# Three weight products of a MoE by Strassen's algorithm, in a kernel of attention and two MoEs

## The chip, the cores and the metric

One core of a Trainium2 chip. The metric is the device time of one execution in microseconds, as the median of several.

## The reference

```python
# attention: q, k, v of (4, 8, 576, 64); a banded and a downsampled softmax attention, summed
x = attn_out.transpose(0, 2, 1, 3).reshape(2304, 512)
h = x @ w_in                                   # first MoE, d_ff 2048
x = (h * np.clip(h + 3.0, 0.0, 6.0) / 6.0) @ w_out
h = np.maximum(np.maximum(x @ w1, x @ w2), x @ w3)   # second MoE, d_ff 768
return h @ w_out2                              # (2304, 512), float32
```

## The kernel before

The attention works on 16 pairs of heads (4 batches times 4 pairs). Pairs 4 to 15 are spread over the steps of the first MoE: `FIRST` (L145) gives the half-step at which each begins, and the last one ends at half-step 92, which is step 46.

Every product of the MoEs is made of three matmuls (`three`, L686): an operand is split into a high part (rounded to the matmul's format by a ScalarE copy) and a low part (operand minus high, by VectorE or GpSimd), and high x high, high x low and low x high are added in PSUM.

The first MoE takes the 2304 tokens in chunks of 512, 512, 512, 512 and 256 (`E1`, L126) and d_ff in 16 blocks of 128, which makes 80 steps; step s is chunk s // 16, block s % 16. In step s TensorE runs `hidden(s + 1)` (12 matmuls into bank 3) and then `add_out(s)` (12 matmuls into four banks). ScalarE and VectorE take each hidden block through `gate_relu`, `gate`, `gate_high` and `gate_low` (L1093, L1380, L1102, L1387). All engines run one program written out in order: what stands behind a waiting instruction on its engine waits with it. `hidden(s)` waits for `gate(s - 1)`, since there is one bank; `add_out(s)` waits for `gate_low(s)`. At a chunk's end `copy_y` (L1108 ScalarE, L1394 VectorE) takes the four result banks to y, and `store_y` (L482) sends y to a scratch tensor in HBM; the next chunk's first `add_out` waits for `copy_y`, bank by bank.

The second MoE has the same chunks (`E2`, L133). `load_xr` (L488) fetches a chunk of x, and `split_x2` (L1114, L1400) splits it, for chunk 0 in steps 56 to 59. A step `hidden2(e, f)` (L871) makes the three products of one block of 128 of the d_ff, 36 matmuls into three banks; there are two sets of three banks. `act_step2` (L1209) and `dve_step2` (L1469) take the maximum of the three and split it into hs. After a chunk's six steps `out2` (L966) multiplies hs with the last weight, 18 matmuls of 512 columns for each tile of 128 tokens, and `copy_out` (L1225) and a store take the result away. The four weights are loaded by `load_w2` (L498) into the places of the first MoE's weights, one after the other as its last chunk (steps 64 to 79) frees them, and split there by `high_w2` (L1125, ScalarE) and by GpSimd's subtraction (L678). Two thirds of `hidden2(0, 0)` stand ahead of `add_out(79)`, and the last third behind it.

DMAs are issued on SyncE's queue, in the order written, each behind its own waits.

## Time and profile before

| | |
|---|---|
| median of 3 runs | 809.03 us (808.30 to 810.23) |
| the profiled execution | 810.8 us, span 809.0 us |
| TensorE busy | 793.4 us, 98% of the span |
| VectorE, ScalarE, GpSimd busy | 314.1, 277.3, 164.1 us |
| HBM traffic | 38.79 MB read, 9.44 MB written |

The span runs from the first to the last instruction. A busy TensorE means that matmuls are in flight; they are pipelined, so one of 0.39 us may start 0.23 us after the one before it. The distance between two starts (the pitch) is therefore what a matmul costs in a stream. A view of groups says how long an instruction takes; the timeline says when it starts and, in brackets, for how long its engine was idle and what ended that.

### The profile page before, as it was taken

The page shows a single profiled execution, that of the slowest core. Times are in us where ns is not written, and L with a number is a line of the kernel's source. Part 1 is how long each engine was busy: PE and PEld are TensorE (multiplying, and loading weights), DVE is VectorE, ACT ScalarE, POOL GpSimd, SP SyncE. Part 2 cuts the span into 40 slices and gives each one's busy share as a digit, 9 for nine tenths or more (in the row PEclk, how much of TensorE's full clock was granted, in tenths as well). Part 3 has the DMA queues.
Part 4 walks back from the last instruction along what each step waited for, and adds up shares of the span by engine and source line. Part 5 has one row for each costly group of instructions (what it writes and reads, how often), then busy time and mean ns, then how long its engine had stood idle before and what let it go on. Part 6 is the DMA issues. An engine that isn't in the chain of part 4 may idle for free.

```text
span 809.0 us, 12700 instructions
## 1 busy us (share of the span) xinstructions
PE 793.4 (98%) x5344; PEld 659.0 (81%) x5344; DVE 314.1 (39%) x602; ACT 277.3 (34%) x619; POOL 164.1 (20%) x196
## 2 busy tenths in 40 slices
PE   7889999999999999999999999999999999999998
PEld 5667877888787878788888899888888888888897
DVE  5864556355444554553323334232123123112211
ACT  4745555343343434433223256221112112111111
POOL 7855756221022102210000048100000000000000
PEclk9999999999999999999999999999999999999999
DMA  8982412221211321110200066100110020010010
GB/s 176 207 260 69 113 48 61 57 79 39 62 39 32 103 62 32 30 32 30 76 1 0 1 196 188 61 0 1 53 52 1 36 70 0 14 66 0 14 40 27
DMA packets 93477, 49.06 MB, mean 61 GB/s; under 512 B 61164, under 2 KB 84204, under 8 KB 93420
## 3 DMA queue, kind: packets, MB, share of 16 engines
q1 hardware_dynamic: 90740, 47.36, 21.3%
q10 hardware_dynamic: 2680, 0.89, 0.6%
q8 instruction: 42, 0.69, 0.4%
q14 instruction: 15, 0.12, 0.1%
HBM read 38.79 MB, written 9.44 MB: 60 GB/s over the span
## 4 chain that ended last, share of the span: by engine, by line
PE 93%; POOL 2%; DVE 2%; ACT 1%; DMA 1%; SPq 1%; issue 1%; DVEq 0%; POOLq 0%
PE bank L688 29%; PE bank L690 28%; PE bank L689 28%; PE bank L823 1%; PE bank L800 1%; PE bank L745 1%; PE bank L789 1%; PE bank L762 1%; DMA k_nat_c<-in_k_dram 1%; PE bank L775 1%; POOL w L641 1%; PE bank L707 1%; POOL dp_a L633 1%; PE bank L717 1%; SPq L415 0%
## 5 line engine op out<-in xcount | busy, mean ns | idle before, releaser
L688 PE MATMUL bank<-xs,w 128*128 128x512 f32 (+1 forms) x680 | 253.5, 373 | 1.1 <-DVE xs L1356 1.0
L689 PE MATMUL bank<-xs,w 128*128 128x512 f32 (+1 forms) x680 | 250.5, 368 | 0.0
L690 PE MATMUL bank<-xs,w 128*128 128x512 f32 (+1 forms) x680 | 250.4, 368 | 0.0
L688 PEld LDWEIGHTS bank<-xs,w 128*128 128x128 f32 x680 | 128.4, 189 | 23.4 <-POOL w L641 1.4
L690 PEld LDWEIGHTS bank<-xs,w 128*128 128x128 f32 x680 | 128.3, 189 | 21.7
L689 PEld LDWEIGHTS bank<-xs,w 128*128 128x128 f32 x680 | 128.4, 189 | 20.4
L688 PE MATMUL bank<-gs,w 128*128 128x512 f32 (+1 forms) x320 | 121.6, 380 | 0.0
L1384 DVE SCALAR_TENSOR_TENSOR rg<-rg,bank 128x512 f32<-128x512 f32 (+1 forms) x80 | 50.7, 634 | 177.3 <-ACT rg L1100 177.3
L689 PE MATMUL bank<-gs,w 128*128 128x512 f32 (+1 forms) x320 | 118.1, 369 | 0.0
L690 PE MATMUL bank<-gs,w 128*128 128x512 f32 (+1 forms) x320 | 118.0, 369 | 0.0
L1100 ACT ACTIVATE rg<-bank,half 128x512 f32<-128x512 f32 (+1 forms) x80 | 51.6, 646 | 177.8 <-PE bank L690 177.8
L1391 DVE TENSOR_TENSOR gs<-rg,gs 128x512 fp32r<-128x512 f32 (+1 forms) x80 | 61.6, 770 | 39.2 <-ACT gs L1106 39.1
L1474 DVE TENSOR_TENSOR hm<-hm,bank 128x512 f32<-128x512 f32 (+1 forms) x30 | 19.0, 635 | 136.9 <-ACT hm L1215 136.9
L688 PEld LDWEIGHTS bank<-gs,w 128*128 128x128 f32 x320 | 60.3, 188 | 12.0 <-issue 1.9
L690 PEld LDWEIGHTS bank<-gs,w 128*128 128x128 f32 x320 | 60.3, 189 | 10.5
L689 PEld LDWEIGHTS bank<-gs,w 128*128 128x128 f32 x320 | 60.4, 189 | 8.9
L1215 ACT ACTIVATE hm<-bank 128x512 f32<-128x512 f32 (+1 forms) x30 | 16.7, 555 | 140.1 <-PE bank L690 140.1
L1106 ACT ACTIVATE gs<-rg 128x512 fp32r<-128x512 f32 (+1 forms) x80 | 47.3, 591 | 31.3 <-DVE rg L1384 31.3
L641 POOL TENSOR_TENSOR w<-w_raw,w 128x256 fp32r<-128x256 f32 x64 | 47.2, 768 | 28.4 <-ACT w L1072 28.4
L678 POOL TENSOR_TENSOR w<-w_raw,w 128x1024 fp32r<-128x1024 f32 x12 | 28.9, 2411 | 116.3 <-ACT w L1128 116.3
L1479 DVE TENSOR_TENSOR hs<-hm,hs 128x512 fp32r<-128x512 f32 (+1 forms) x30 | 19.2, 639 | 79.4 <-ACT hs L1223 79.4
L623 POOL TENSOR_TENSOR lp_a<-lp_a,linv_a 128x320 f32<-128x320 f32 x28 | 20.2, 741 | 145.8 <-DVE linv_a L1323 145.8
(211 smaller groups left out, 822.5 us busy)
## 6 DMA issues: line engine op xcount, KB each, us to landing
w_raw<-in_moe_w_out_dram SPq DMA_DIRECT2D x22, 256.0 KB, 4.8
w_raw<-in_moe_w_dram SPq DMA_DIRECT2D x18, 256.0 KB, 3.2
out_dram<-o_sb SPq DMA_DIRECT2D x18, 256.0 KB, 2.0
w_raw<-in_moe_w_in_dram SPq DMA_DIRECT2D x16, 256.0 KB, 3.9
x_scratch<-y SPq DMA_DIRECT2D x4, 1024.0 KB, 4.8
xr<-x_scratch SPq DMA_DIRECT2D x4, 1024.0 KB, 6.4
q_nat_a<-in_q_dram SPq DMA_DIRECT2D x26, 144.0 KB, 2.8
v_a<-in_v_dram SPq DMA_DIRECT2D x24, 144.0 KB
```

The costliest lines, as they stand in the source:

```text
L623: mine = g.tensor_tensor(lp[:, a:b], lp[:, a:b], t.linv[:, a:b].unsqueeze(2).to_broadcast([P, b - a, KW]), ALU.mult)
L641: mine = g.tensor_tensor(w1[:, f, 1, 2 * i:2 * i + 2], w1_raw[f][:, 2 * i:2 * i + 2], w1[:, f, 0, 2 * i:2 * i + 2].bitcast(F32), ALU.subtract)
L678: g.tensor_tensor(w2[:, m, 1], w2_raw[m][:], w2[:, m, 0].bitcast(F32), ALU.subtract).then_inc(s_w2, 1)
L688: mm(dst, w[0], m[0], start=start, stop=False, skip_group_check=True)
L689: mm(dst, w[0], m[1], start=False, stop=False, skip_group_check=True)
L690: return mm(dst, w[1], m[0], start=False, stop=stop, skip_group_check=True)
L1100: fn(gated(s), hidden_bank(s)[:, 0:n], ACT.Relu, bias=half[:, 0:1], scale=1.0 / 6.0).then_inc(s_relu, 1)
L1106: fn(gs[:, s % 2, 0, 0:n], gated(s), ACT.Copy).then_inc(s_gh, 1)
L1384: vec.scalar_tensor_tensor(out=gated(s), in0=gated(s), scalar=1.0, in1=hidden_bank(s)[:, 0:n], op0=ALU.min, op1=ALU.mult).then_inc(s_g, 1)
L1391: vec.tensor_tensor(gs[:, s % 2, 1, 0:n], gated(s), gs[:, s % 2, 0, 0:n].bitcast(F32), ALU.subtract).then_inc(s_gl, 1)
L1474: vec.tensor_tensor(got, got, bank[HBANK[f % 2][1]][:, 0:n], ALU.max).then_inc(s_m1, 1)
L1479: vec.tensor_tensor(hs[:, f, 1, 0:n], got, hs[:, f, 0, 0:n].bitcast(F32), ALU.subtract).then_inc(s_hl, 1)
```

## The change

The tokens of the second MoE are taken in three chunks of 768, and each of its three weights in three pieces of 256 columns (a pair of d_ff blocks). A block is one piece of one weight: a product of (768 x 512) with (512 x 256). Cut in two along each dimension it has eight products of quarters; Strassen's algorithm in Winograd's form has seven, of 384 tokens by 256 by 128, with four sums on either side and seven afterwards. Four sums of the weights' quarters (`sum_block`, VectorE), their high and low parts (`high_block` on ScalarE, `low_block` on GpSimd) are made after steps 47, 52, 53, 55, 56, 58, 59, 61 and 62 of the first MoE (`READY`) and stored to a new HBM tensor t2, 1.8 MB for each of nine blocks. There is one landing place b_raw for the weights and two sets of ph and pl for their parts. SyncE loads block b + 1 when block b's copies of b_raw are made, then stores block b. In the second MoE the blocks come back through a ring of four places, four of them (the last of the chunk before, in reversed order) without a load in chunks 1 and 2. The sums of x are made by `sum_x2`, `high_x2` and `low_x2`: for chunk 0 in steps 71 to 75, for the others during `out2`. Of the seven products, some are added up in PSUM (two banks take products 0 and 3 or 1 and 4, the third 2 and 5; product 6 takes the first again); the rest is added by VectorE, and one sum by GpSimd. The last weight is loaded and split by itself (`load_wo`, `high_wo`, `low_wo`).

The diff, cut to its core:

```diff
-    E2 = [0, 512, 1024, 1536, 2048, 2304]
-    NC2 = len(E2) - 1
-    N2 = [b - a for a, b in zip(E2, E2[1:])]
-    CH2 = max(N2)
-    T2 = [n // P for n in N2]
...
+    NC2 = 3
+    E2 = TOK // NC2
+    N2 = E2 // 2
+    T2 = E2 // P
+    PAIRS2 = F2 // 2
...
+    ORDER = [list(range(BLOCKS))[::1 - 2 * (e % 2)] for e in range(NC2)]
...
+    PRODUCTS = [0, 4, 3, 1, 5, 2, 6]
+    NPR = len(PRODUCTS)
+    RING = 4
...
+    LOADS = [(e, j) for e in range(NC2) for j in range(0 if e == 0 else RING, BLOCKS)]
...
+        READY = {47: 0, 52: 1, 53: 2, 55: 3, 56: 4, 58: 5, 59: 6, 61: 7, 62: 8}
+        BANKS2 = [[5, 6, 7], [0, 1, 2]]
...
+            def load_block(b):
+                if b == 0:
                     sp.wait_ge(s_x, 2 * NP)
                 else:
-                    sp.wait_ge(s_x2l, KT * e)
-                done = next(c for c in range(NC1) if E1[c + 1] >= E2[e + 1]) + 1
-                sp.wait_ge(s_ys, 16 * done)
-                sp.dma_start(xr[:, :, 0:N2[e]], x1[:, :, E2[e]:E2[e + 1]]).then_inc(s_xr, 16)
-            def load_w2(m):
-                sp.wait_ge(s_o, F1 * (NC1 - 1) + m + 1)
+                    sp.wait_ge(s_t, 4 * b)
+                    sp.wait_ge(s_th, 3 * b)
+                    sp.wait_ge(s_tl2, NPR * (b - 1) + 3)
+                sp.dma_start(b_raw[:].rearrange("p i k f c -> p (i k) (f c)"),
+                             w2_v[b % 3][b // 3]).then_inc(s_braw, 16)
+            def store_block(b):
+                sp.wait_ge(s_tl2, NPR * (b + 1))
+                for j, part_of in enumerate((ph, pl)):
+                    sp.dma_start(t2[b, :, j, :], part_of[b % 2][:].rearrange("p o k c -> p (o k c)").bitcast(F32)).then_inc(s_ts[b % 2], 16)
+            def load_xr(e):
+                if e:
+                    sp.wait_ge(s_xol, NPR * e)
+                done = next(c for c in range(NC1) if E1[c + 1] >= E2 * (e + 1)) + 1
+                sp.wait_ge(s_ys, 16 * max(done, NC1 - 1))
+                sp.dma_start(xr[:], x1[:, :, E2 * e:E2 * (e + 1)]).then_inc(s_xr, 16)
...
+            def load_wo(f):
                 for i in range(2):
-                    sp.dma_start(w2_raw[m][:, i * KT:(i + 1) * KT, :],
-                                 w2_v[2 * (m % 2) + i][m // 2]).then_inc(s_w2raw[m], 16)
+                    sp.wait_ge(s_ts[i], 32 * ((BLOCKS + 1 - i) // 2))
+                sp.dma_start(wo_raw[f][:], wo_v[f]).then_inc(s_wo[f], 16)
+            def load_wt(e, j):
+                b = ORDER[e][j]
+                i = b % RING
+                if j < RING:
+                    sp.wait_ge(s_o, F1 * (NC1 - 1) + NPR + 2 * i + 2)
+                else:
+                    sp.wait_ge(s_pr, NPR * (block2(e, j)[0] - RING + 1))
+                sp.wait_ge(s_ts[b % 2], 32 * (b // 2 + 1))
+                sp.dma_start(wt[i][:, :, 0:NPR].rearrange("p j o k c -> p j (o k c)").bitcast(F32), t2[b]).then_inc(s_wt[i], 16)
...
+            load_block(0)
             store_y(2)
+            for b in range(BLOCKS):
+                if b + 1 < BLOCKS:
+                    load_block(b + 1)
+                store_block(b)
+            store_y(3)
             load_xr(0)
-            store_y(3)
-            for m in range(2 * F2):
-                load_w2(m)
+            for f in range(F2):
+                load_wo(f)
+            for j in range(RING):
+                load_wt(0, j)
             load_xr(1)
...
             store_y(4)
+            for j in range(RING, BLOCKS):
+                load_wt(0, j)
             for e in range(NC2):
-                if e >= 1 and e + 1 < NC2:
-                    load_xr(e + 1)
-                for m in range(T2[e]):
-                    sp.wait_ge(s_oc, tile0(e) + m + 1)
...
+            def low_block(b):
+                high, low = ph[b % 2], pl[b % 2]
+                if b >= 2:
+                    pool.wait_ge(s_ts[b % 2], 32 * (b // 2))
+                for o, raw in enumerate((b_raw[:, 0, :, 0], b_raw[:, 1, :, 0], b_raw[:, 1, :, 1])):
+                    pool.wait_ge(s_th, 3 * b + 1 + o // 2)
+                    g.tensor_tensor(low[:, o], raw, high[:, o].bitcast(F32), ALU.subtract).then_inc(s_tl2, 1)
+                pool.wait_ge(s_t, 4 * b + 4)
+                pool.wait_ge(s_th, 3 * b + 3)
+                for o in range(3, NPR):
+                    g.tensor_tensor(low[:, o], pl_sum[b % 2][:, o], high[:, o].bitcast(F32),
+                                    ALU.subtract).then_inc(s_tl2, 1)
+            for b in range(BLOCKS):
+                low_block(b)
...
+            def sum_c22(e, j):
+                t, i, w = block2(e, j)
+                pool.wait_ge(s_v, t + 1)
+                pool.wait_ge(s_p5, t + 1)
+                if j % 3 == 0:
+                    if t:
+                        pool.wait_ge(s_hl, 4 * (t // 3 - 1) + 2)
+                    g.tensor_tensor(hm[3], v_t[:], p5[:], ALU.add).then_inc(s_c22, 1)
+                else:
+                    g.tensor_tensor(p5[:], v_t[:], p5[:], ALU.add).then_inc(s_add, 1)
+            for e in range(NC2):
+                for j in range(BLOCKS):
+                    sum_c22(e, j)
+                    if e == 0 and 1 <= j < 1 + F2:
+                        low_wo(j - 1)
...
+            def product(e, j, i):
+                t, _, _ = block2(e, j)
+                b = ORDER[e][j]
+                if j == 0:
+                    pe.wait_ge(s_xol, NPR * e + i + 1)
+                if i == 0:
+                    pe.wait_ge(s_wt[b % RING], 16 * loads_of(e, j))
+                    if t >= 2:
+                        pe.wait_ge(s_c21, t - 1)
+                    if t == 1:
+                        pe.wait_ge(s_yv, 2 * NC1)
+                        pe.wait_ge(s_ya, 2 * NC1)
+                if i == 3:
+                    pe.wait_ge(s_p1, t + 1)
+                if i == 4:
+                    pe.wait_ge(s_u2, t + 1)
+                if i == 5:
+                    pe.wait_ge(s_p5, t + 1)
+                if i == 6:
+                    pe.wait_ge(s_c11, t + 1)
+                dst = bank[BANKS2[t % 2][i % 3]][:, 0:N2]
+                for kk in range(2):
+                    mine = three(dst, [wt[b % RING][:, h, PRODUCTS[i], kk, :] for h in range(2)],
+                                 [xo[i][:, h, kk, :] for h in range(2)],
+                                 kk == 0 and i in (0, 1, 2, 6), kk == 1)
+                mine.then_inc(s_pr, 1)
             def add_out(s):
...
                 add_out(s)
                 attend(2 * s + 1)
-            OBANK = [4, 7]
...
-                    if m == 0 or f0:
-                        pe.wait_ge(s_hl, F2 * e + f + 1)
-                    whi, wlo = (w2[:, 2 * f + 1, j, KT:2 * KT, :].rearrange("p a b -> p (a b)") for j in range(2))
-                    mine = three(bank[OBANK[i % 2]][:], [hs[:, f, j, m * P:(m + 1) * P] for j in range(2)],
-                                 [whi, wlo], f == 0, f == F2 - 1)
-                if f1 == F2:
+                for at in range(a, b):
+                    pe.wait_ge(s_hl, 4 * (PAIRS2 * e + at) + 3 + (at < PAIRS2 - 1 or m >= T2 // 2))
+                    if e == 0:
+                        pe.wait_ge(s_wol, F2)
+                    pair = ORDER[e][3 * at] // 3
+                    for x in range(2):
+                        mine = three(bank[OBANK[i % 2]][:], [hs[pair][:, x, h, m * P:(m + 1) * P] for h in range(2)],
+                                     [wo[:, 2 * pair + x, h] for h in range(2)], at == 0 and x == 0,
+                                     at == PAIRS2 - 1 and x == 1)
+                if b == PAIRS2:
                     mine.then_inc(s_o2, 1)
-            hidden2(0, 0, (0,))
-            pe.wait_ge(s_yv, 2 * NC1)
-            pe.wait_ge(s_ya, 2 * NC1)
+            for i in range(3, NPR):
+                product(0, 0, i)
             for e in range(NC2):
-                for f in range(1, F2):
-                    hidden2(e, f)
...
-                    for m in range(T2[e]):
-                        out2(e, m, 0, F2 - 1)
-                    for m in range(T2[e]):
-                        out2(e, m, F2 - 1, F2)
+                for j in range(0 if e else 1, BLOCKS):
+                    for i in range(NPR):
+                        product(e, j, i)
+                for m in range(2):
+                    out2(e, m, 0, PAIRS2 - 1)
+                for m in range(2):
+                    out2(e, m, PAIRS2 - 1, PAIRS2)
+                for m in range(2, T2):
+                    out2(e, m, 0, PAIRS2)
...
+            def high_block(b):
+                high, low = ph[b % 2], pl_sum[b % 2]
+                act.wait_ge(s_braw, 16 * (b + 1))
+                if b >= 2:
+                    act.wait_ge(s_ts[b % 2], 32 * (b // 2))
+                fn(high[:, 0:2], b_raw[:, :, :, 0], ACT.Copy).then_inc(s_th, 1)
+                fn(high[:, 2], b_raw[:, 1, :, 1], ACT.Copy).then_inc(s_th, 1)
+                act.wait_ge(s_t, 4 * b + 4)
+                fn(high[:, 3:NPR], low[:, 3:NPR], ACT.Copy).then_inc(s_th, 1)
+            def high_x2(e, i):
+                if i == 0:
                     act.wait_ge(s_xr, 16 * (e + 1))
-                if e == 1:
-                    act.wait_ge(s_ys, 16 * (NC1 - 1))
-                if e >= 2:
-                    act.wait_ge(s_h2, F2 * (e - 1))
-                fn(xs2[e % 2][:, 0, kk, 0:N2[e]], xr[:, kk, 0:N2[e]], ACT.Copy).then_inc(s_x2h, 1)
...
-                act.wait_ge(s_w2raw[m], 32)
-                fn(w2[:, m, 0], w2_raw[m][:], ACT.Copy).then_inc(s_w2h, 1)
+                if e:
+                    act.wait_ge(s_pr, NPR * BLOCKS * e)
+                else:
+                    act.wait_ge(s_o, F1 * (NC1 - 1) + i + 1)
+                if i in (1, 2, 4, 5):
+                    act.wait_ge(s_s, 4 * e + {2: 1, 1: 2, 4: 3, 5: 4}[i])
+                    src = xo_sum[i][:]
+                else:
+                    src = {0: xr[:, 0:2, 0:N2], 3: xr[:, 2:4, 0:N2], 6: xr[:, 2:4, N2:E2]}[i]
...
-                if c == NC1 - 2 and 8 <= f < 12:
-                    split_x2(0, f - 8)
-                if c == NC1 - 1 and 2 <= f < 2 + 2 * F2:
-                    high_w2(f - 2)
+                if s in READY:
+                    high_block(READY[s])
+                if c == NC1 - 1 and 7 <= f < 11:
+                    for i in range(NPR)[2 * (f - 7):2 * (f - 6)]:
+                        high_x2(0, i)
                 if f == F1 - 1:
...
-                for f in range(F2):
-                    act_step2(e, f)
-                    if 1 <= f < 5 and e + 1 < NC2:
-                        split_x2(e + 1, f - 1)
-            copy_out(NC2 - 1)
+                for j in range(BLOCKS):
+                    copy_p1(e, j)
+                    if j and j % 3 == 0:
+                        high_h(e, j - 1, 3)
+                        high_h(e, j - 1, 1)
+                    copy_p5(e, j)
+                    if j and j % 3 == 0:
+                        high_h(e, j - 1, 2)
+                    if j % 3 == 2:
+                        high_h(e, j, 0)
+                    if e == 0 and j < F2:
+                        high_wo(j)
+                for which in (3, 1, 2):
+                    high_h(e, BLOCKS - 1, which)
...
+            def sum_block(b):
+                low = pl_sum[b % 2]
+                dve.wait_ge(s_braw, 16 * (b + 1))
+                if b >= 2:
+                    dve.wait_ge(s_ts[b % 2], 32 * (b // 2))
+                t1, t2, t3, t4 = (low[:, 3 + i] for i in range(4))
+                b11, b12, b21, b22 = (b_raw[:, i, :, j] for i in range(2) for j in range(2))
+                vec.tensor_tensor(t1, b12, b11, ALU.subtract).then_inc(s_t, 1)
+                vec.tensor_tensor(t3, b22, b12, ALU.subtract).then_inc(s_t, 1)
+                dve.wait_ge(s_t, 4 * b + 1)
+                vec.tensor_tensor(t2, b22, t1, ALU.subtract).then_inc(s_t, 1)
+                dve.wait_ge(s_t, 4 * b + 3)
+                vec.tensor_tensor(t4, b21, t2, ALU.subtract).then_inc(s_t, 1)
...
+            def sum_x2(e):
+                dve.wait_ge(s_xr, 16 * (e + 1))
...
+                    dve.wait_ge(s_pr, NPR * BLOCKS * e)
+                else:
+                    dve.wait_ge(s_o, F1 * (NC1 - 1) + NPR)
+                s2, s1, s3, s4 = (xo_sum[i][:] for i in (1, 2, 4, 5))
+                a11, a12, a21, a22 = (xr[:, j:j + 2, i * N2:(i + 1) * N2] for i in range(2) for j in (0, 2))
+                vec.tensor_tensor(s1, a21, a22, ALU.add).then_inc(s_s, 1)
+                dve.wait_ge(s_s, 4 * e + 1)
+                vec.tensor_tensor(s2, s1, a11, ALU.subtract).then_inc(s_s, 1)
+                vec.tensor_tensor(s3, a11, a21, ALU.subtract).then_inc(s_s, 1)
+                dve.wait_ge(s_s, 4 * e + 2)
+                vec.tensor_tensor(s4, a12, s2, ALU.subtract).then_inc(s_s, 1)
...
+            def low_x2(e, i):
+                dve.wait_ge(s_xoh, NPR * e + i + 1)
+                if i in (1, 2):
+                    dve.wait_ge(s_s, 4 * e + 4)
+                src = {0: xr[:, 0:2, 0:N2], 3: xr[:, 2:4, 0:N2], 6: xr[:, 2:4, N2:E2]}.get(i)
+                src = xo_sum[i][:] if src is None else src
+                vec.tensor_tensor(xo[i][:, 1], src, xo[i][:, 0].bitcast(F32), ALU.subtract).then_inc(s_xol, 1)
...
+                if s in READY:
+                    sum_block(READY[s])
+                if c == NC1 - 1 and f == 7:
+                    sum_x2(0)
+                if c == NC1 - 1 and 8 <= f < 12:
+                    for i in range(NPR)[2 * (f - 8):2 * (f - 7)]:
+                        low_x2(0, i)
                 if f == F1 - 1:
...
-                for f in range(F2):
-                    dve_step2(e, f)
-                    if 1 <= f < 5 and e + 1 < NC2:
-                        split_x2(e + 1, f - 1)
+                for j in range(BLOCKS):
+                    take_u2(e, j)
...
+                        low_h(e, j - 1, 3)
+                    take_c11(e, j)
+                    if j and j % 3 == 0:
+                        low_h(e, j - 1, 1)
+                        low_h(e, j - 1, 2)
+                    take_v(e, j)
+                    take_c12(e, j)
+                    if j % 3:
+                        max_c12(e, j)
+                        max_c22(e, j)
+                    take_c21(e, j)
+                    if j % 3:
+                        max_c21(e, j)
+                for which in (0, 3, 1, 2):
+                    low_h(e, BLOCKS - 1, which)
+                if e + 1 < NC2:
+                    sum_x2(e + 1)
+                    for i in range(NPR):
+                        low_x2(e + 1, i)
```

## Rows read from the trace of the kernel before

**Rows 1.** The page: the span, section 1 of TensorE, the granted clock of section 2.
```profile
span 809.0 us, 12700 instructions
...
PE 793.4 (98%) x5344; PEld 659.0 (81%) x5344; DVE 314.1 (39%) x602; ACT 277.3 (34%) x619; POOL 164.1 (20%) x196
...
PEclk9999999999999999999999999999999999999999
```
**Rows 2.** Busy time by stretch: us, PE, PEld, DVE, ACT, POOL (x), PEclk, DMA share, GB/s.
```profile
700.00:740.00 40.00, 40.00 (x178) 33.14 (x177) 6.10 (x11) 6.58 (x12) 0.00 (x0) 1.00 0.12 40
```
**Rows 3.** Timeline of ScalarE, chunk 0 of the second MoE; start us, us, instruction.
```profile
526.97 0.60 ACT L1215 ACTIVATE hm<-bank 128x512 f32<-128x512 f32 x1 [5.45 <-PE bank L690]
...
535.13 0.60 ACT L1215 ACTIVATE hm<-bank 128x512 f32<-128x512 f32 x1 [4.93 <-PE bank L690]
```
**Rows 4.** Timeline of ScalarE, last chunk of the first MoE.
```profile
504.84 0.47 ACT L1100 ACTIVATE rg<-bank,half 128x256 f32<-128x256 f32 x1 [0.55 <-PE bank L690]
...
507.72 0.47 ACT L1100 ACTIVATE rg<-bank,half 128x256 f32<-128x256 f32 x1 [0.55 <-PE bank L690]
```
**Rows 5.** Timeline of TensorE: `hidden(79)`'s last matmul, the second MoE's first and last.
```profile
507.40 0.28 PE L690 MATMUL bank<-xs,w 128*128 128x256 f32 x1
...
508.96 0.40 PE L688 MATMUL bank<-xs,w 128*128 128x512 f32 x1
...
805.46 0.39 PE L690 MATMUL bank<-w,hs 128*128 128x512 f32 x1
```
**Rows 6.** Groups by line and shape (busy us, mean ns, idle before), one timeline row.
```profile
L1479 DVE TENSOR_TENSOR hs<-hm,hs 128x512 fp32r<-128x512 f32 x24 | 16.6, 693 | 61.0 <-ACT hs L1223 61.0
...
L1479 DVE TENSOR_TENSOR hs<-hm,hs 128x256 fp32r<-128x256 f32 x6 | 2.6, 426 | 18.4 <-ACT hs L1223 18.4
...
L1128 ACT ACTIVATE w<-w_raw 128x1024 fp32r<-128x1024 f32 x12 | 12.5, 1044 | 0.1
...
L1223 ACT ACTIVATE hs<-hm 128x512 fp32r<-128x512 f32 x24 | 15.2, 632 | 31.0 <-DVE hm L1476 31.0
...
L1223 ACT ACTIVATE hs<-hm 128x256 fp32r<-128x256 f32 x6 | 2.5, 416 | 4.7 <-DVE hm L1476 4.7
...
L1015 ACT ACTIVATE kT_a<-bank 128x384 f32<-128x384 f32 x14 | 7.0, 501 | 0.0
...
516.06 0.66 ACT L1112 ACTIVATE y<-bank 128x256 f32<-128x256 f32 x2 [6.96 <-PE bank L690]
```
**Rows 7.** Timeline of ScalarE and VectorE, last step of 512 columns.
```profile
459.07 0.69 ACT L1100 ACTIVATE rg<-bank,half 128x512 f32<-128x512 f32 x1 [3.36 <-PE bank L690]
460.51 0.63 ACT L1106 ACTIVATE gs<-rg 128x512 fp32r<-128x512 f32 x1 [0.76 <-DVE rg L1384]
...
459.79 0.69 DVE L1384 SCALAR_TENSOR_TENSOR rg<-rg,bank 128x512 f32<-128x512 f32 x1 [3.36 <-ACT rg L1100]
461.18 0.69 DVE L1391 TENSOR_TENSOR gs<-rg,gs 128x512 fp32r<-128x512 f32 x1 [0.70 <-ACT gs L1106]
```
**Rows 8.** Timeline of GpSimd and VectorE where both work, in the first MoE.
```profile
127.62 2.82 POOL L641 TENSOR_TENSOR w<-w_raw,w 128x256 fp32r<-128x256 f32 x4 [5.74 <-ACT w L1072]
...
134.02 3.95 POOL L641 TENSOR_TENSOR w<-w_raw,w 128x256 fp32r<-128x256 f32 x4 [1.53 <-ACT w L1072]
...
134.76 1.22 DVE L1391 TENSOR_TENSOR gs<-rg,gs 128x512 fp32r<-128x512 f32 x1
...
480.34 1.03 DVE L1391 TENSOR_TENSOR gs<-rg,gs 128x256 fp32r<-128x256 f32 x1 [0.48 <-ACT gs L1106]
...
478.67 2.40 POOL L678 TENSOR_TENSOR w<-w_raw,w 128x1024 fp32r<-128x1024 f32 x1 [0.69 <-ACT w L1128]
```
**Rows 9.** DMA issues (KB each, median us from issue to landing); one stretch of an xr load.
```profile
xr<-x_scratch SPq DMA_DIRECT2D x4, 1024.0 KB, 6.4
...
xr<-x_scratch SPq DMA_DIRECT2D x1, 512.0 KB, 3.9
...
588.00:589.00 1.00, 1.00 (x6) 0.84 (x5) 0.00 (x0) 0.00 (x0) 0.00 (x0) 1.00 1.02 395
```

More of the change, by code:

```diff
@@ L311, in attention_moe_kernel @@
+        hm = [hm_a[:, 0], hm_a[:, 1], hm_b[:, 0], hm_b[:, 1]]
+        hs_at = [xs_at[0], xs_at[0] + 2 * 2 * E2 * 4, M_AT - W_FSZ]
+        hs = [place(hs_at[i], f"hs{i}", [P, 2, 2, E2], F32R) for i in range(PAIRS2)]
+        assert hs_at[1] + 2 * 2 * E2 * 4 <= gs_end and xs_at[1] + 4 * (KT * E2 + 2 * N2) <= xs_at[0]
+        assert hs_at[2] + 2 * 2 * E2 * 4 <= xs_at[1]
         q_v = q.rearrange("b h (j r) d -> b h r j d", j=J)
```

299 lines of the change are left out of this document (193 added, 106 removed).

## The prediction

> **What bounds the kernel now.** I read four views in this order. First the page: TensorE is busy for 98% of the span and its granted clock stands at the full level, 2.4 GHz, in every slice [rows 1]. So the question is what the matmuls cost and whether anything makes them wait. Second, the busy time by stretch: inside the second MoE TensorE is busy 40.00 of 40.00 us while VectorE and ScalarE are busy for about 6 us each [rows 2]. Third, the timeline, for the pitch of one matmul. Two ScalarE evictions of successive steps of the second MoE start 8.16 us apart [rows 3]; a step is 36 matmuls of 512 columns, so one takes 0.2267 us. Two steps of the first MoE's last chunk are 2.88 us apart for 24 matmuls of 256 columns [rows 4], 0.1200 us each. Both lie on one line: 0.0133 us and 0.4167 ns per column (2.4 GHz). For 384 columns, which no row has, the line gives 0.1733 us. Its bounds are 0.170 (proportional to 512) and 0.2267 (no cheaper than 512); I take the line, since two widths lie on it. Fourth, the ends: the second MoE's first matmul starts at 508.96, its last at 805.46 [rows 5]. Counting 1188 matmuls of 512, 216 of 256 and the 12 of the last `add_out` gives 269.3 + 25.9 + 1.4 = 296.6 us; the rows leave 296.5 + 0.2. There is no stall in the second MoE, so each matmul removed is time won and each new wait is time lost.
>
> **What is removed.** The products with three weights are 864 matmuls of 512 and 216 of 256: 195.8 + 25.9 = 221.8 us. After: 3 chunks x 9 blocks x 7 products x 2 x 3 = 1134 of 384 columns, 196.6 us. `out2` stays at 324 of 512. **Gain 25.2 us.**
>
> At this place the Trainium skill, "TensorE: Matmul & The Clock Gate", section "Back-to-back issue gap", speaks against the change: it gives about 131 ns per matmul sustained at 512 columns and 81 ns at 128, so that narrow matmuls cost nearly what wide ones do. Interpolated, an estimate, the gain would be 5 us. The pitches of [rows 3, 4] contradict it.
>
> **Inside the new second MoE.** A product is six matmuls, 1.04 us; a block is 7.28 us. VectorE does up to 8 operations per block and 4 more per pair, 0.56 us each (between 0.426 at 256 and 0.693 at 512 columns, [rows 6]): 4.5 us of 7.28. ScalarE adds two evictions of 0.50 us and GpSimd one sum of about 1.05 us (0.70 per 256 columns, [rows 8]). A result is taken up 0.20 us after its last matmul gives way to the next (507.40 + 0.12, eviction at 507.72; [rows 4, 5]). So p1 is there at 1.8 us and wanted at 3.1; u2 at 2.9, wanted at 4.2; p5 at 3.9, wanted at 5.2; c11 at 5.0, wanted at 6.2. VectorE's last maximum ends near 9.4 and the next block's u2 can start at 9.6. Every margin is over 1 us, so I cost these waits at nothing; if VectorE fell behind by 1.3 us per block it would be the bound. A block's weights are 1.8 MB; at the 395 GB/s of a full stretch [rows 9] that is 4.7 us plus a start of about 1.4, and only five loads per chunk fall into 58 us. Nothing.
>
> Four places are not covered:
> - Start: ScalarE must copy y(4) (0.66 us for two, [rows 6]) after the last `add_out`, then p1, before product 3: 0.2 + 0.66 + 0.5 = **1.4 us**. Before, `hidden2` covered this.
> - Ends of chunks 0 and 1: `copy_out(e,0)` stands behind `high_x2` 1 and 2, which wait for VectorE's sums, which stand behind four `low_h`. I get the copy at 15.9 us after the last product, against TensorE's 15.4: 0.5 us, twice, **1.0 us**.
> - The first chunk's operands, made in steps of 2.88 us. At f = 7 VectorE runs four sums of 768 columns (0.96 each by the line through [rows 6]) after `gate_low`, ending at 5.5 us, so the gate ends at 5.9 where `hidden` wants it at 4.1: 1.9. Then three steps with two `low_x2` take VectorE 3.2 us of 2.88: 0.9. **2.8 us.** GpSimd is idle then.
> - The weights' sums, made at the listed steps of the first MoE, 5.44 us each.
>
> **The weights' sums** are the large term. A step's chain begins with `gate_relu`; from it to the end of `gate_high` are 2.07 us and to the end of `gate_low` 2.80 (459.07, 460.51, 459.79, 461.18 and their lengths, [rows 7]). `high_block` and `sum_block` stand behind these, and the next `gate_relu` stands behind `high_block` on ScalarE. `hidden(s+2)` can begin 2.72 us after `hidden(s+1)` ends and wants the gate; with 0.69 + 0.03 + 0.69 + 0.05 us for relu and gate, `gate_relu` may be 1.06 us late at no cost. The last action of `high_block` (1024 columns, 1.05 us, [rows 6]) waits for VectorE's four dependent sums.
>
> Those compete with GpSimd's lows. The trace: four GpSimd subtractions take 2.82 us alone, but 3.95 when VectorE starts operations with two SBUF inputs beside them, one of which takes 1.22 us instead of 0.69; and a VectorE subtraction of 256 columns takes 1.03 instead of 0.43 when a GpSimd one of 2.40 is under way, ending with it [rows 8]. So they take turns. This is the rule of the Trainium skill, "SBUF — State Buffer", section "Who interferes with whom": a shared port, held for a whole instruction, and the loser blocks. By that rule the sum is the one below; without it, it is the first rival.
>
> First block of a pair (steps 52, 55, 58, 61), from relu = 0: GpSimd and VectorE alternate from 2.8 (0.67 and 0.30), the sums end at 6.2, `high_block` at 7.3; relu and gate end at 8.7 against 7.96: **0.8 us**. Only then is b_raw free. Its next load of 512 KB in 1 KB pieces takes 3.9 us like the xr load of that size [rows 9]: landed at 11.3. The second block (steps 53, 56, 59, 62) follows one step behind, so ScalarE sits in `high_block` with `gate_relu` behind it: two copies (0.63 + 0.4, [rows 6]), the sums and the last copy end 3.3 to 3.9 after landing, at 14.9; the gate at 16.35 against 14.2: **2.15 us**. Three pairs: **8.9**. The fourth runs into the 256-column chunk: 0.8 + 2.9, and 0.5 more because `copy_y(3)` is late: **4.2**. Block 0 at step 47 delays `copy_y(2)`: sums end at 6.2, the first copy at 6.9, `add_out(48)` wants it at 5.24, and ScalarE's copy adds 0.3: **1.9**. Bounds of this group (15.0): 8 (no turns, sums end early) and 25 (the load takes 6.4 us like the 1 MB one, four times 2.5 more).
>
> Each of some 17 stalls also shows a weight load that was hidden; loads are busy 659.0 us in 5344 [rows 1], 0.12 each: **2.0 us**. Removed work (`high_w2`, GpSimd's part of it, `split_x2`) lay beside TensorE and gives nothing.
>
> Sum: -25.2 + 1.4 + 1.0 + 2.8 + 15.0 + 2.0 = -3.0 us. The profiled execution took 810.8 (span 809.0), 1.8 above the median of 809.03; so 807.8 in a like execution, **806.0 us** as a median. A difference under 0.2% (1.6 us) can't be told from none.
>
> **Rivals.**
> 1. The cover holds better: VectorE's sums are not held up by GpSimd. Then first blocks cost nothing, second ones 1.4, the group 8: 799. For: the order of turns is only seen in few rows, and the first two sums may precede GpSimd's. Against: [rows 8]. Chance 0.25. That nearly no stall appears (786) has 0.05: it needs b_raw to land 3 us sooner than any such load here.
> 2. Slower: the reload of b_raw. It is issued alone and its landing decides four times. At 4.65 us instead of 3.9 the gain is gone; at 6.4, the 1 MB row, it is 10 us worse: 816. Against: stores of the block before are done by then by my count. Chance 0.15.
> 3. The new phase is bound by the blocks' weights: by the slope between the xr loads of 512 KB and 1 MB (3.9 and 6.4 us, [rows 9]) a block takes 10.1 us, more than its 7.28, and chunk 0, where nine must come, would lose about 5 us: 811. Against: the stretch with 395 GB/s. Chance 0.07.
> 4. It does not cut TensorE's time as counted: a 384-column matmul costs 0.20 us, halfway to the upper bound. Then 1134 x 0.027 = 30 us go, and 836 results. Against: the line through two widths. Chance 0.03. The interpolated rule of the Trainium skill's page on TensorE, above, is of this kind and would give about 826.
> The forecast keeps 0.45, its own range 802 to 810.
>
> **The numbers.** Range 795 to 814: it takes in the forecast, rival 1, rival 3 and half of rival 2. Faster: 0.27 of the forecast's 0.45, and 0.30, makes 0.57. Same: 0.13 and 0.05, 0.18. Slower: 0.25.
>
> **What would show it.** Evictions of the second MoE 7.28 us apart per block and matmuls of 384 columns 0.173 apart; in the list of waits TensorE waiting in the first MoE for the gate (VectorE), about 2 us at a time, with ScalarE's `high_block` waiting for the b_raw load just before; VectorE's sums of 256 columns lasting 0.7 to 0.8 us. If `gate_relu` of steps 55, 58 and 61 starts on time, the large term is wrong. If TensorE waits inside blocks for u2 or c11, or for weights by DMA, my margins are wrong.

## The result, and the profile after

The changed kernel takes **798.51 us** (median of four runs, 797.5 to 799.76), the kernel before 809.63 beside it (808.3 to 812.01): ratio 0.9867, 95% interval 0.9851 to 0.9883. The profiled execution took 799.48 us. It is faster, as forecast, and clear of the spread, but by 11 us and not by 3. The time lies inside the stated range of 795 to 814, close to rival 1's 799 and not to the forecast's 806.

The page of the kernel after, cut:

```profile
span 797.7 us, 13594 instructions
...
PE 773.2 (97%) x5398; PEld 668.3 (84%) x5398; DVE 414.9 (52%) x786; ACT 299.5 (38%) x671; POOL 221.7 (28%) x280
...
wt<-t_scratch SPq DMA_DIRECT2D x19, 1792.0 KB, 7.6
...
b_raw<-in_moe_w_dram SPq DMA_DIRECT2D x9, 512.0 KB, 3.8
```

Against [rows 1] TensorE is busy 20.2 us less in 54 matmuls more, and VectorE 101 us more. TensorE is still the bound; the question is how long it waits. Its list of waits (what was waited for: us in total, times, longest):

```profile
PE bank L841 <- DVE rg L1587: 7.1, 7, 1.8
...
PE bank L841 <- DVE y L1601: 1.3, 1, 1.3
PE bank L841 <- ACT p L1392: 1.2, 1, 1.2
```

The first is the gate of the first MoE, late seven times; the second is `copy_y(2)` at step 48; the third is the first product's copy when the second MoE starts. Nothing in the second MoE waits for a DMA or for VectorE. The timeline of TensorE shows its matmuls' pitch and two of the stalls:

```profile
420.64 0.50 PE L841 MATMUL bank<-xs,w 128*128 128x512 f32 x1 [1.16 <-DVE rg L1587]
...
474.43 0.39 PE L841 MATMUL bank<-xs,w 128*128 128x256 f32 x1 [1.83 <-DVE rg L1587]
...
521.31 0.34 PE L841 MATMUL bank<-xo,wt 128*128 128x384 f32 x1
521.48 0.34 PE L842 MATMUL bank<-xo,wt 128*128 128x384 f32 x1
...
794.15 0.39 PE L843 MATMUL bank<-wo,hs 128*128 128x512 f32 x1
```

A matmul of 384 columns starts 0.17 us after the one before. From 521.31 to 794.15 + 0.23 are 273.1 us, where the kernel before needed 296.7 [rows 5]: **23.6 us** won in the second MoE. By count it is 1134 x 0.1733 + 324 x 0.2267 + 1.4 (the last `add_out`) = 271.4; the wait at the start, another 1.4 us, and 0.3 of small gaps are the rest. In the timeline of ScalarE the blocks' first evictions stand 7.28 us apart, as counted:

```profile
532.72 0.49 ACT L1392 ACTIVATE p<-bank 128x384 f32<-128x384 f32 x1 [4.72 <-PE bank L843]
...
540.00 0.49 ACT L1392 ACTIVATE p<-bank 128x384 f32<-128x384 f32 x1 [4.19 <-PE bank L843]
```

**What the stalls cost.** For each stall I take the distance between two matmuls' starts less the pitch of their width, from TensorE's timeline. After 366 us, where the weights' sums begin, the kernel before loses 0.3 us so; the changed one:

| place | forecast | measured |
|---|---|---|
| block 0, step 48 | 1.9 | 1.5 |
| three first blocks of a pair | 2.4 | 0.9 |
| three second blocks | 6.45 | 3.7 |
| ahead of the 256-column chunk | 4.2 | 2.3 |
| chunk 0's operands | 2.8 | 2.1 |
| start of the second MoE | 1.4 | 1.4 |
| chunk ends | 1.0 | 0 |
| restarts, other small gaps | 2.0 | 1.3 |
| half clock behind one stall | 0 | 1.7 |
| sum | 22.2 | 14.9 |

A stall's restart is inside "measured" where it shows in the first gap; the second matmul comes another 0.1 us late, which the line on restarts holds. The gain of 25.2 less 14.9, with the 0.3 us of the kernel before, is 10.6. The profiled difference is 810.8 − 799.48 = 11.3, and 1.0 us of it is a first MoE that reached step 48 sooner, which differs between executions (375.2 to 377.8 us over ten profiles of these kernels). That leaves 10.3 for the change, so the table accounts for it within 0.3 us.

One pair of blocks, in the timeline of four engines, shows where the stall at 420.64 comes from:

```profile
405.40 0.69 ACT L1260 ACTIVATE rg<-bank,half 128x512 f32<-128x512 f32 x1 [3.06 <-PE bank L843]
...
411.33 1.06 ACT L1285 ACTIVATE ph<-pl_sum 128x1024 fp32r<-128x1024 f32 x1 [3.03 <-DVE pl_sum L1618]
412.30 0.67 ACT L1260 ACTIVATE rg<-bank,half 128x512 f32<-128x512 f32 x1
...
416.22 0.63 ACT L1281 ACTIVATE ph<-b_raw 128x512 fp32r<-128x512 f32 x1 [1.87 <-DMA b_raw<-in_moe_w_dram]
...
418.23 1.06 ACT L1285 ACTIVATE ph<-pl_sum 128x1024 fp32r<-128x1024 f32 x1 [1.07 <-DVE pl_sum L1618]
419.20 0.67 ACT L1260 ACTIVATE rg<-bank,half 128x512 f32<-128x512 f32 x1
...
408.12 0.97 DVE L1613 TENSOR_TENSOR pl_sum<-b_raw 128x256 f32<-128x256 f32 x1
409.01 0.95 DVE L1614 TENSOR_TENSOR pl_sum<-b_raw 128x256 f32<-128x256 f32 x1
409.89 0.95 DVE L1616 TENSOR_TENSOR pl_sum<-b_raw,pl_sum 128x256 f32<-128x256 f32 x1
410.88 0.42 DVE L1618 TENSOR_TENSOR pl_sum<-b_raw,pl_sum 128x256 f32<-128x256 f32 x1
...
416.22 0.43 DVE L1613 TENSOR_TENSOR pl_sum<-b_raw 128x256 f32<-128x256 f32 x1 [1.02 <-DMA b_raw<-in_moe_w_dram]
...
417.36 0.84 DVE L1618 TENSOR_TENSOR pl_sum<-b_raw,pl_sum 128x256 f32<-128x256 f32 x1
...
408.07 2.49 POOL L798 TENSOR_TENSOR pl<-b_raw,ph 128x256 fp32r<-128x256 f32 x3 [21.66 <-ACT ph L1281]
...
417.00 2.50 POOL L798 TENSOR_TENSOR pl<-b_raw,ph 128x256 fp32r<-128x256 f32 x3 [1.19 <-ACT ph L1281]
...
412.48 0.38 SPq L568 DMA_DIRECT2D b_raw<-in_moe_w_dram  x1
```

First block: `gate_relu` starts at 405.40. While GpSimd makes its three lows (408.07 to 410.56), VectorE's sums of 256 columns last 0.95 to 0.97 us; the fourth, with GpSimd done, 0.42. ScalarE waits 3.03 us in the middle of `high_block` for them, and the next `gate_relu` (412.30) is that late. Second block: the load goes out at 412.48, since it waits for all three copies of the first block, and lands at 416.22; ScalarE stands in `high_block` again, the next `gate_relu` can't start before 419.20, and TensorE stalls at 420.64. That is the forecast's chain. It is shorter than forecast because in the second block GpSimd begins 0.8 us after the landing and only the last sum is held up.

### The profile page after: what moved, and what is told of

Read it like the earlier page. It is cut to its first block, busy times and chain, and to the rows that moved or that the text cites. A ratio compares the mean times of both kernels' runs of the same rounds, so it can differ in the third digit from the quotient of the medians.

```text
span 797.7 us, 13594 instructions
## 1 busy us (share of the span) xinstructions
PE 773.2 (97%) x5398; PEld 668.3 (84%) x5398; DVE 414.9 (52%) x786; ACT 299.5 (38%) x671; POOL 221.7 (28%) x280
## 4 chain that ended last, share of the span: by engine, by line
PE 83%; DVE 5%; ACT 3%; POOL 3%; DMA 2%; SPq 2%; issue 2%; DVEq 0%; POOLq 0%
PE bank L841 26%; PE bank L843 25%; PE bank L842 25%; DMA b_raw<-in_moe_w_dram 2%; PE bank L976 1%; PE bank L953 1%; PE bank L898 1%; POOL w L755 1%; DVE rg L1587 1%; ACT rg L1260 1%; PE bank L942 1%; DVE pl_sum L1618 1%; PE bank L915 1%; PE bank L928 1%; DVE pl_sum L1616 1%
## 5 line engine op out<-in xcount | busy, mean ns | idle before, releaser
L841 PE MATMUL bank<-xs,w 128*128 128x512 f32 (+1 forms) x320 | 122.8, 384 | 8.2 <-DVE rg L1587 7.1
L841 PE MATMUL bank<-xo,wt 128*128 128x384 f32 x378 | 126.4, 334 | 1.2 <-ACT p L1392 1.2
L843 PE MATMUL bank<-xo,wt 128*128 128x384 f32 x378 | 126.3, 334 | 0.0
L842 PE MATMUL bank<-xo,wt 128*128 128x384 f32 x378 | 126.3, 334 | 0.0
L843 PE MATMUL bank<-xs,w 128*128 128x512 f32 (+1 forms) x320 | 118.6, 371 | 0.0
L842 PE MATMUL bank<-xs,w 128*128 128x512 f32 (+1 forms) x320 | 118.5, 370 | 0.0
L841 PEld LDWEIGHTS bank<-xs,w 128*128 128x128 f32 x320 | 60.7, 190 | 23.3 <-DVE rg L1587 10.2
L1594 DVE TENSOR_TENSOR gs<-rg,gs 128x512 fp32r<-128x512 f32 (+1 forms) x80 | 57.8, 723 | 39.2 <-ACT gs L1266 39.1
L841 PEld LDWEIGHTS bank<-xo,wt 128*128 128x128 f32 x378 | 70.9, 188 | 1.5 <-issue 1.4
L842 PEld LDWEIGHTS bank<-xo,wt 128*128 128x128 f32 x378 | 71.0, 188 | 0.1
L843 PEld LDWEIGHTS bank<-xo,wt 128*128 128x128 f32 x378 | 70.9, 188 | 0.0
L843 PEld LDWEIGHTS bank<-xs,w 128*128 128x128 f32 x320 | 60.7, 190 | 10.5
L842 PEld LDWEIGHTS bank<-xs,w 128*128 128x128 f32 x320 | 61.0, 190 | 9.0
```

What stands on the lines that cost most here:

```text
L841: mm(dst, w[0], m[0], start=start, stop=False, skip_group_check=True)
L842: mm(dst, w[0], m[1], start=False, stop=False, skip_group_check=True)
L843: return mm(dst, w[1], m[0], start=False, stop=stop, skip_group_check=True)
L1594: vec.tensor_tensor(gs[:, s % 2, 1, 0:n], gated(s), gs[:, s % 2, 0, 0:n].bitcast(F32), ALU.subtract).then_inc(s_gl, 1)
```

## The experiments

The question after the result is what the remaining 15 us hang on. **Theory A**: the reload of b_raw lands too late. **Theory B**: GpSimd and VectorE take turns, and ScalarE waits for the held-up sums. In the trace both stand in the same chain. The kernel before took 809.50 us beside the runs with the second b_raw, the load sooner, the wait on GpSimd and the one block, and 810.08 beside the others, so a difference of medians from the two groups is uncertain by some 0.6 us.

**A second b_raw**, loads two blocks ahead:

```diff
+        b_raws = [b_raw, work("b_raw1", [P, 2, 2, 2, P])]
...
-                else:
+                elif b >= 2:
-                    sp.wait_ge(s_t, 4 * b)
+                    sp.wait_ge(s_t, 4 * (b - 1))
...
-                if b + 1 < BLOCKS:
-                    load_block(b + 1)
+                if b + 2 < BLOCKS:
+                    load_block(b + 2)
```

> The landing place b_raw is doubled, so that a block's load is issued two blocks ahead. Theory A (the second block of a pair is late because ScalarE waits 1.8 us for b_raw's reload): the three stalls of 1.1 to 1.3 us and most of the one of 2.0 us before the 256-column chunk go; about 5 us less than the changed kernel, near 793.5. Theory B (VectorE and GpSimd take turns at a shared port): VectorE's sums can start 1 us sooner, but then each of the four meets GpSimd's subtractions of the block before and of its own and takes 0.95 us instead of 0.43, so they end no sooner; within 1 us of the changed kernel, near 798, with sums of 0.95 us in the trace.

Measured: 802.39 us, ratio to before 0.9903 [0.9886, 0.9921]: 4 us **slower** than the change as it was. Neither theory had that: A put it at 793.5, B at 798. Its list of waits has the gate late for longer:

```profile
PE bank L844 <- DVE rg L1591: 9.4, 7, 2.4
```

VectorE's timeline in the second block of the same pair:

```profile
416.23 0.96 DVE L1618 TENSOR_TENSOR pl_sum<-b_raw 128x256 f32<-128x256 f32 x1
...
418.98 0.84 DVE L1623 TENSOR_TENSOR pl_sum<-b_raw,pl_sum 128x256 f32<-128x256 f32 x1
```

The data is there; now the sums start while GpSimd is at its lows, and last 0.96, 0.96, 0.95 and 0.84 instead of 0.43, 0.42, 0.42 and 0.84. Counted from the `gate_relu` ahead of them (413.40 here, 412.30 in the change) the sums start 1.1 us sooner (at 2.83 and not 3.92) and end 0.5 us later (at 6.42 and not 5.90). The stall of a second block grows from 1.25 to 1.84 us. So B had the mechanism, and only its size too small.

**The same load, released one copy sooner** (ScalarE's last copy reads the sums, not b_raw):

```diff
-                    sp.wait_ge(s_th, 3 * b)
+                    sp.wait_ge(s_th, 3 * b - 1)
```

> The reload of b_raw waits for the two copies that read it and no longer for the third, which reads the sums: it is issued about 1.1 us sooner. If the second blocks' stalls are set by the landing (A), each of the three shrinks from about 1.25 to about 0.2 us and the last from 2.0 to 0.9: about 4.4 us less, near 794. If they are set by the turns of VectorE and GpSimd (B), the sums start sooner but meet GpSimd's last four subtractions of the block before (until 415.8 in the changed kernel's profile, the landing would be at 415.1): 1 to 2 us less, near 797.

Measured: 801.01 us, 0.9891 [0.9871, 0.9911], 2.5 us slower, where A had 794 and B 797. This interval overlaps the change's own (0.9851 to 0.9883); the profile says the same as the median, with 13.5 us of gaps against 11.6. The timelines of SyncE, VectorE and GpSimd:

```profile
410.08 0.38 SPq L568 DMA_DIRECT2D b_raw<-in_moe_w_dram  x1
...
413.88 0.96 DVE L1613 TENSOR_TENSOR pl_sum<-b_raw 128x256 f32<-128x256 f32 x1
...
416.63 0.84 DVE L1618 TENSOR_TENSOR pl_sum<-b_raw,pl_sum 128x256 f32<-128x256 f32 x1
...
411.29 3.27 POOL L804 TENSOR_TENSOR pl<-pl_sum,ph 128x256 fp32r<-128x256 f32 x4 [1.97 <-ACT ph L1285]
414.63 2.56 POOL L798 TENSOR_TENSOR pl<-b_raw,ph 128x256 fp32r<-128x256 f32 x3
```

Against ScalarE's last copy of the first block (410.09 here, 411.33 in the change) the load goes out 1.2 us sooner and the sums begin 1.1 us sooner (3.79 us behind it, not 4.89). They fall into the 3.27 us in which GpSimd still makes the block before, and then beside its three lows. The turns take back more than the landing gives: their four lengths are 3.7 us here and 2.1 in the change. Theory A alone is refuted twice: an earlier landing makes the stalls longer. Theory B's forecast of a small gain is missed too, since it counted the turns with the block before and not those with the block's own three lows.

**GpSimd's lows behind the sums**, one wait more on GpSimd:

```diff
+                pool.wait_ge(s_t, 4 * b + 4)
                 for o, raw in enumerate((b_raw[:, 0, :, 0], ...
```

> One wait more: GpSimd's first three subtractions of a block wait until VectorE's four sums of that block are made. Theory B (turns): all four sums take 0.43 us, they end 1.4 us sooner in first blocks and 0.4 in second ones; first-block stalls (0.24 to 0.39) go, the one at step 48 shrinks by 1.3, second ones by 0.8 each; about 5 us less, near 793.5. Theory A (only the reload counts): GpSimd's third subtraction, which frees b_raw, comes later or at the same time, so nothing is gained: 798 to 799.

Measured: 794.19 us, 0.9812 [0.9797, 0.9827], 4.3 us faster than the change. Its list of waits has the gate late five times, not seven:

```profile
PE bank L842 <- DVE rg L1588: 5.7, 5, 1.6
```

The timelines of VectorE (second block), GpSimd (first block) and SyncE:

```profile
414.11 0.43 DVE L1614 TENSOR_TENSOR pl_sum<-b_raw 128x256 f32<-128x256 f32 x1 [1.97 <-DMA b_raw<-in_moe_w_dram]
...
415.24 0.43 DVE L1619 TENSOR_TENSOR pl_sum<-b_raw,pl_sum 128x256 f32<-128x256 f32 x1
...
408.06 2.14 POOL L799 TENSOR_TENSOR pl<-b_raw,ph 128x256 fp32r<-128x256 f32 x3 [21.96 <-DVE pl_sum L1619]
...
410.30 0.38 SPq L568 DMA_DIRECT2D b_raw<-in_moe_w_dram  x1
```

No engine does less; it is the order. The four sums last 0.42 to 0.43 us each, GpSimd's three lows 2.14 instead of 2.49. The stall at step 48 and the three at first blocks are gone (2.4 us), the seconds fall from 1.25 to 1.0. What is left of them is the landing: the load goes out at 410.30, behind the lows that now come later, and lands at 414.11.

**Both**, the second b_raw and the wait:

> GpSimd's wait together with the doubled b_raw, which alone made it slower. Theory B (turns): now the second block's sums meet only GpSimd's last four subtractions of the block before, two sums take about 0.9 us and two 0.43, and they end 1 us sooner than with the wait alone; second-block stalls of 1.0 us go, the last one (1.75) shrinks to 0.7: about 790. Theory A (reload) by itself expects the same here, but did not expect the doubled b_raw alone to be slower. If the four late subtractions hold up all four sums, it is no faster than the wait alone: 794.

Measured: 790.23 us, 0.9757 [0.9741, 0.9773]. With the turns out of the way the second b_raw is worth 4.0 us, where it cost 3.9 without. Its list of waits shows the gate late twice, ahead of the 256-column chunk and at chunk 0's operands, and no more in any pair of the 512-column chunks:

```profile
PE bank L845 <- DVE rg L1592: 2.2, 2, 1.5
```

VectorE's first two sums of a second block still last 0.95 us there, beside GpSimd's four lows of the block before (409.67 to 413.13), but now they start early enough. So the two waits cover each other, and each theory is right about what is left once the other's wait is gone.

**One block instead of nine.** This kernel makes block 0's weights' sums only and reads them for all nine blocks, so eight of its nine blocks have the wrong weights:

```diff
-        READY = {47: 0, 52: 1, 53: 2, 55: 3, 56: 4, 58: 5, 59: 6, 61: 7, 62: 8}
+        READY = {47: 0}
...
-            for b in range(BLOCKS):
-                low_block(b)
+            low_block(0)
```

> Only block 0 of the weights' sums is made and stored, and the second MoE reads it for all nine: blocks 1 to 8 are left out. The stalls counted from the matmuls' starts say what they cost: 0.9 (first blocks) + 3.7 (second ones) + 2.3 (before the 256-column chunk) and up to 1.7 where the granted clock fell to half for 3.4 us: 7 to 9 us less, 790 to 791.5. If the eight blocks also cost something that those stalls do not show (traffic that slows the matmuls, a later start of the weights' loads), it is more than 9.

Measured: 790.63 us, 0.9762 [0.9747, 0.9777]. The eight blocks cost 7.9 us, all that they do to the second MoE's loads included; by the table they are 0.9 + 3.7 + 2.3 of stalls, restarts, and at times the clock. Step 48, the operands and the start stay (1.5, 1.7, 1.4). The kernel with both waits removed reaches 790.23 while it makes all nine.

**The three places outside the sums.** ScalarE's first product copy ahead of `copy_y(4)`; at step 47 `copy_y(2)` ahead of `high_block` and `sum_block`; VectorE's four sums of chunk 0 split over steps 71 and 72 and its `low_x2` over five steps, and ScalarE's `high_x2` over five steps and not four:

```diff
+                if s in READY and f == F1 - 1:
+                    copy_y(c)
                 if s in READY:
                     high_block(READY[s])
...
+                if s == STEPS - 1:
+                    copy_p1(0, 0)
...
-                if c == NC1 - 1 and f == 7:
-                    sum_x2(0)
+                if c == NC1 - 1 and f in (7, 8):
+                    sum_x2(0, f - 7)
```

> Three changes of place, nothing else: p1 of block 0 is copied ahead of y(4) on ScalarE; chunk 0's sums of x are made two per step (steps 71 and 72) and their low parts up to step 77, not four sums in one step; at step 47 both engines copy y(2) ahead of block 0 of the weights' sums. If the stalls of 1.38, 1.71 and 1.54 us stand for themselves, they go and the time falls by about 4.5 us, to 794. Rival: a stall taken away is given back by the next thing that is late (block 0's load or the low parts for product 6), and less than 2.5 us is gained.

Measured: 795.82 us, 0.9827 [0.9813, 0.9842], 2.7 us faster than the change, between the expected 4.5 and the rival's 2.5. The operands' stall is gone (1.7), the start falls from 1.38 to 0.52 and waits for VectorE's u2 now. At step 48 the copy is on time and the stall only moves: ScalarE's `high_block` now ends later, the gate of the next step with it (0.91 instead of 1.54).

**That order with the wait on GpSimd**, and **all three**:

> The three changes of place, and GpSimd's first three subtractions behind VectorE's sums. The waits lie at different places: 794.2 (GpSimd's wait alone) less 1.4 and 1.7, the one at step 48 being gone already: about 791. Rival: block 0 now ends later than before at step 48 and delays step 49: 793.

> Everything together: GpSimd's wait, doubled b_raw, three changes of place. No stall over 0.3 us is left but about 0.7 ahead of the 256-column chunk: 13.2 of the counted 15 us (and the fallen clock) are won back at the most; about 787, near the 786 that the count of matmuls alone gives. Rival: the doubled b_raw gives nothing beside GpSimd's wait: 791.

Measured: 791.93 us, 0.9778 [0.9763, 0.9792], and **787.80 us, 0.9729 [0.9715, 0.9744]** (787.35 to 789.12). The latter beats both kernels: 10.7 us below the change, 22.3 below the kernel before beside it. Its page:

```profile
span 786.1 us, 13596 instructions
...
PE 770.2 (98%) x5398; PEld 667.0 (85%) x5398; DVE 411.2 (52%) x786; ACT 300.0 (38%) x671; POOL 219.0 (28%) x280
```

From 366 us on its list of waits holds one late gate, the start and a wait for `copy_y(3)`:

```profile
PE bank L845 <- DVE rg L1597: 0.7, 1, 0.7
...
PE bank L845 <- DVE u L1738: 0.4, 1, 0.4
...
PE bank L845 <- DVE y L1611: 0.3, 1, 0.3
```

In gaps of over 0.12 us it loses 2.0 us there, of 25.2 that the removed matmuls give. The stalls and the medians, side by side:

| kernel | us | step 48 | first | second | 256 chunk | operands | start | gaps after 366 us |
|---|---|---|---|---|---|---|---|---|
| the change | 798.51 | 1.5 | 0.9 | 3.7 | 2.3 | 1.7 | 1.4 | 11.6 |
| second b_raw | 802.39 | 1.5 | 0.9 | 5.5 | 2.9 | 1.7 | 1.4 | 14.0 |
| load sooner | 801.01 | 1.5 | 0.9 | 5.6 | 2.4 | 1.7 | 1.4 | 13.5 |
| wait on GpSimd | 794.19 | 0 | 0 | 3.0 | 2.2 | 1.7 | 1.4 | 8.3 |
| order | 795.82 | 0.9 | 0.9 | 4.1 | 2.6 | 0 | 0.5 | 9.1 |
| wait, order | 791.93 | 0 | 0 | 2.7 | 2.2 | 0 | 0.5 | 5.4 |
| wait, second b_raw | 790.23 | 0 | 0 | 0 | 1.3 | 1.7 | 1.4 | 4.4 |
| all three | 787.80 | 0 | 0 | 0.1 | 1.3 | 0 | 0.5 | 2.0 |

The last column sums the gaps over 0.12 us, without the clock; chunk 0's operands are 1.7 here and 2.1 above, where the small gaps behind the long one count too. Medians and stalls agree step by step: the wait on GpSimd 3.3 us in gaps and 4.3 in the median (its profile has the full clock behind the stall ahead of the 256-column chunk, 1.00 from 470 to 476 us, where the change's fell), the second b_raw on top of it 3.9 and 4.0, the order on top of both 2.4 and 2.4.

## Why the prediction was right or wrong

The step that failed is the size of the weights' sums, the large term of the sum: 15.0 us forecast, 8.4 measured, 6.6 too many. Restarts (2.0 against 1.3), the chunk ends (1.0 against 0) and chunk 0's operands (2.8 against 2.1) were too large as well, 2.4 us together; a fall of the clock that the sum didn't have took 1.7 back. So the losses were 14.9 and not 22.2, against a gain that was right: 10.3 us are left where the forecast had 3, and the first MoE that came 1.0 us sooner makes it 11. The mechanism of the term holds, as the wait on GpSimd and the second b_raw show; what failed in it is how long the chain takes.

**The gain: right.** 25.2 us rested on the line through two widths; 384 columns have the pitch that it gives, 0.173 us, and blocks stand 7.28 apart. Rival 4 falls. The Trainium skill, "TensorE: Matmul & The Clock Gate", section "Back-to-back issue gap", gives about 0.131 us a matmul sustained at 512 columns, by which the estimated gain was 5 us. The traces contradict it, with 0.227 us at 512 columns and 0.173 at 384.

**Inside the second MoE: right.** No wait for u2, p5, c11 or a block's weights. The weights' loads take 7.6 us where the text had 4.7 plus 1.4, so that term was too small; against five loads in a chunk of 58 us it doesn't show: TensorE never waits for one. Rival 3, which had 10.1 us a load, falls with it.

**The start: right** (1.4 forecast, 1.38 measured), and the cure confirms what it waited for.

**The chunk ends: wrong, 1.0 us that isn't there.** The forecast had the copy at 15.9 against TensorE's 15.4. (It says "after the last product", but both figures count from the start of the last block, here 582.44.) ScalarE's row shows it from 14.4 to 15.0 us:

```profile
596.87 0.58 ACT L1424 ACTIVATE o_sb<-bank 128x512 f32<-128x512 f32 x1
```

The step that failed here is the price of the operations: I added whole lengths (0.56, 0.96). In a row of operations one starts before the last one's length is over: here the sums of 0.95 us stand 0.87 apart and operations on 384 columns, 0.55 long, 0.47; the sums at 409.01 and 409.89 above do the same. (A sum that needs the result of the one before comes later: 0.99 us here.) A length is what one operation takes, a pitch is what it costs in a row. I had used the pitch for the matmuls and the length for everything else.

**Chunk 0's operands: right place, 2.8 against 2.1.** The long stall is 1.7 where 1.9 stood; the three later steps cost some 0.1 us each and not 0.3, for the same reason.

**The weights' sums: right chain, size off by 6.6 us** (15.0 forecast, 8.4 measured, inside the bounds of 8 and 25). Block 0 is 0.4 of it, and three steps of the sum did the rest. (1) First blocks: relu and gate were put 0.8 us late; the sums ended at 5.9 us and `high_block` at 7.0, not 6.2 and 7.3, and 0.3 was left. (2) Second blocks: the load takes 3.7 us against 3.9, and with the sooner release it lands at 10.8 and not 11.3. But from the landing to the end of the last copy I had 3.3 to 3.9 and took the middle. Only the last of the four sums is held up, since GpSimd begins 0.8 us after the landing. It is 3.1 (416.22 to 419.29), `gate_relu` comes at 13.8 instead of 14.9, and the stall is 1.25 instead of 2.15. (3) Ahead of the 256-column chunk 2.3 instead of 4.2: each piece as in (1) and (2), and the 0.5 for `copy_y(3)` didn't appear. (With the wait on GpSimd it does: TensorE's first `add_out` of that chunk is 0.46 us late for VectorE's y.)

**Restarts: too large.** 0.12 us for each of 17 stalls stood there; some ten stalls came, each with 0.1 us at its second matmul.

**Rival 1**, "VectorE's sums are not held up", gave 799 and the time is 798.5. The time was met and the reason was not: in the changed kernel the sums of every first block are held up. The experiment with the wait on GpSimd is the case that rival 1 described, and it takes 794. What helped the number is that in second blocks three of the four sums come ahead of GpSimd's lows, as the rival said two might. Its group of 8 us has no stall in first blocks and 1.4 us in second ones, the measured 8.4 has 0.3 and 1.25. That the time then fell on 799 is luck: the terms outside the group were 2.4 us too large, and the clock, which no term had, took 1.7. A number that fits is no proof of its mechanism. The taking of turns is the rule that the prediction drew from the Trainium skill, "SBUF — State Buffer", section "Who interferes with whom"; the trace agrees with it: 0.95 us beside GpSimd, 0.43 without. The order that avoids most of it is worth 4.3 us of the kernel's time. One of its rows was read loosely: the subtraction that starts at 480.34 [rows 8] ends 0.3 us behind GpSimd's (481.37 and 481.07) and not with it.

**Rival 2**, the reload: its landing takes 3.7 to 3.8 us, so it didn't turn the sign. The forecast said that b_raw is free only when `high_block` ends. The changed kernel does wait so, but b_raw is free one copy sooner, as the experiment with the sooner load used; and that an earlier landing would help, which the rival took as plain, is wrong while the engines take turns.

**Not foreseen: the clock**, 1.7 us in the profiled execution (below).

## What to carry to other kernels

When a wait ends a chain, look at what starts if it ends sooner: two engines that block each other can make an earlier transfer cost time, and two waits that cover each other give nothing or less than nothing when one is removed alone. Order the side work so that the engine on whose result another one waits goes first, even at the price of an extra wait on the idle engine. In a sum, use the pitch at which operations follow each other, not the length of one.
